# Products on zeros in the attention preamble, v loaded in turn with q and k, and two product blocks begun on four of six chunks

## What is computed

```python
scores = scale * np.matmul(q_c, k_c.transpose(0, 1, 2, 4, 3))
attn = np.exp(scores - np.max(scores, axis=-1, keepdims=True))
attn = attn / (np.sum(attn, axis=-1, keepdims=True) + 1e-09)
out = np.matmul(attn, v_c)

h = x @ w_in                    # x: 4608 x 512, w_in: 512 x 2048
r = np.maximum(h, 0.0)
g = s * (r * r) + b
x2 = g @ w_out                  # 4608 x 512

e_idx = np.argmax(xc @ w_gate, axis=1)          # xc: rows with x2 @ w_skip > 0
h = np.maximum(xc[mask] @ w1[e], 0.0)           # for each of 8 experts
y[mask] = gate_w[mask, None] * (h @ w2[e])
out[do_compute] = xc + y
```

## Time and profile before

| | |
|---|---|
| time, median of 3 runs | 1368.41 us (1366.62 to 1368.72) |
| the profiled execution's own time | 1368.54 us |
| its span | 1366.6 us |
| TensorE busy over the span | 1334.4 us (98%) |
| TensorE's clock, mean over the span | 0.984 of full |
| VectorE, ScalarE, GpSimd busy | 928.3, 753.6, 310.6 us |
| bytes moved | 116.88 MB, 86 GB/s on average |

### The profile page before, as it was taken

The page is one execution under the profiler, slowest core; times in us unless marked ns, Lnnn a source line. Parts: engine busy times, 40 slices in busy tenths (PEclk is TensorE's granted clock), DMA queues, the critical chain, the costliest instruction groups (busy, mean ns, idle before and its releaser), DMA issues.

```text
span 1366.6 us, 22444 instructions
## 1 busy us (share of the span) xinstructions
PE 1334.4 (98%) x7031; PEld 1175.5 (86%) x7032; DVE 928.3 (68%) x2139; ACT 753.6 (55%) x1838; POOL 310.6 (23%) x274
## 2 busy tenths in 40 slices
PE   8999999999999999999999999999799999999998
PEld 7998989899998999889998999989677778888886
DVE  3786978788786978778796878874477673333332
ACT  3886657566674757566665666644266552222221
POOL 4542222121222312121222222101111111111111
PEclk6999999999999999999999999999899999999999
DMA  6522312031131202112130303042375641111110
GB/s 243 171 82 96 102 32 94 25 101 40 39 97 29 97 30 96 35 59 78 34 103 21 105 24 101 12 155 70 118 255 205 238 156 46 38 45 40 45 38 26
DMA packets 61583, 116.88 MB, mean 86 GB/s; under 512 B 11848, under 2 KB 20296, under 8 KB 61360
## 3 DMA queue, kind: packets, MB, share of 16 engines
q1 hardware_dynamic: 42048, 76.39, 17.1%
q10 hardware_dynamic: 13328, 25.69, 5.4%
q0 software_dynamic: 6112, 13.56, 3.2%
HBM read 91.28 MB, written 27.08 MB: 87 GB/s over the span
## 4 chain that ended last, share of the span: by engine, by line
PE 88%; DVE 5%; issue 4%; DMA 1%; ACT 1%; DVEq 1%; ACTq 0%; SPq 0%; POOLq 0%; POOL 0%
PE h_ps L694 29%; PE y_ps L709 28%; PE y_ps L798 10%; PE h_ps L785 10%; PE s_ps L659 3%; PE av_ps L675 3%; DVE weights_lo L1128 2%; PE t_ps L666 1%; PE t_ps L778 1%; PE s_ps L792 1%; PE av_ps L792 1%; DMA first_raw<-in_first_qk 1%; PE y_ps L649 0%; PE av_ps L649 0%; DVE rows_t_lo L1253 0%
## 5 line engine op out<-in xcount | busy, mean ns | idle before, releaser
L1155 DVE CUSTOM_DVE_ANT_0 products<-scratch,wide 128x512 f32<-128x512 f32 x297 | 287.4, 968 | 6.7
L694 PE MATMUL h_ps<-rows_t_hi,weights_lo 128*128 128x384 f32 x768 | 261.1, 340 | 8.2 <-issue 5.5
L941 ACT ACTIVATE scratch<-h_ps 128x384 f32<-128x384 f32 x192 | 94.5, 492 | 301.9 <-PE h_ps L694 300.0
L694 PE MATMUL h_ps<-rows_t_hi,weights_hi 128*128 128x384 f32 x768 | 260.0, 339 | 0.0
L694 PE MATMUL h_ps<-rows_t_lo,weights_hi 128*128 128x384 f32 x768 | 258.8, 337 | 0.0
L709 PE MATMUL y_ps<-weights_hi,g_lo 128*128 128x512 f32 x576 | 227.9, 396 | 0.3 <-DVE g_lo L1134 0.2
L709 PE MATMUL y_ps<-weights_lo,g_hi 128*128 128x512 f32 x576 | 226.4, 393 | 0.0
L709 PE MATMUL y_ps<-weights_hi,g_hi 128*128 128x512 f32 x576 | 225.9, 392 | 0.0
L1134 DVE TENSOR_TENSOR g_lo<-scratch,g_hi 128x384 fp32r<-128x384 f32 x192 | 120.1, 626 | 102.0 <-ACT g_hi L873 99.4
L694 PEld LDWEIGHTS h_ps<-rows_t_hi,weights_lo 128*128 128x128 f32 x768 | 145.0, 189 | 21.6 <-issue 7.2
L515 POOL TENSOR_TENSOR qk_lo<-qk_raw,qk_hi 128x768 fp32r<-128x768 f32 x66 | 125.2, 1896 | 144.5 <-ACT qk_hi L873 144.5
(11 more groups left out here) (177 smaller groups left out, 2381.6 us busy)
## 6 DMA issues: line engine op xcount, KB each, us to landing
qk_raw<-in_qk SPq DMA_DIRECT2D x66, 384.0 KB, 3.0
expert_raw<-in_w ACTq DMA_DIRECT2D x31, 512.0 KB, 4.4
out<-scratch SPq DMA_DIRECT2D x12, 768.0 KB, 3.8
x_rows<-scratch SPq DMA_DIRECT2D x12, 768.0 KB, 6.0
scratch<-in_w ACTq DMA_DIRECT2D x18, 512.0 KB, 5.9
v_raw<-in_v SPq DMA_DIRECT2D x66, 128.0 KB, 2.0
expert_raw<-in_w SPq DMA_DIRECT2D x12, 512.0 KB, 4.9
wide<-in_w_out SPq DMA_DIRECT2D x7, 512.0 KB, 4.6
```

The costliest lines, as they stand in the source:

```text
L694: mm = pe.matmul(h_ps[f % 2][:, 0:TOK], w[:, f // PAIR, kt, fs], x[:, z, kt, :], start=kt == 0 and n == 0, stop=kt == KT - 1 and n == 2)
L941: act.activation(r_buf[f % 2], h_ps[f % 2][:, 0:TOK], ACT.Relu).then_inc(r_done, 1)
L1155: dve.tensor_tensor_reduce(products[:, :], x2_sb[:, t, :], gate_w[:, e, :], 1.0, 0.0, ALU.mult, ALU.add, logits[:, t, e:e + 1]).then_inc(d ...
```

## The change

Four edits, all of them ahead of or in the first step of the first tile. Products on zeros (now written to `h_ps[1]`) are put between the small products: one after B of chunk 0, three each after B of chunks 1 and 2, and one after D of chunks 0 to 3, 11 in all. The loads of v are issued in turn with those of q and k. The blocks h(0) and h(1) of the first tile are each made in two parts: columns 0 to 255 (chunks 0 to 3, FIRST_PART) while the last two chunks are still in their attention, columns 256 to 383 afterwards. And the preamble's last two steps are written out by hand around these parts.

```diff
+        FIRST_PART = (CPT - 2) * CHUNK
...
-            for c in range(CPT // 2):
-                load_first_qk(c)
+            load_first_qk(0)
+            load_first_qk(1)
             load_first_v(0)
-            load_raw_after(0)
-            for c in range(1, CPT // 2):
-                load_first_qk(c + 2)
+            for c in range(1, CPT - 1):
+                load_first_qk(c + 1)
                 load_first_v(c)
-            load_raw_after(1)
-            load_first_qk(CPT - 1)
-            for c in range(CPT // 2, CPT):
-                load_first_v(c)
-            load_raw_after(2)
+                if c >= 2:
+                    load_raw_after(c - 2)
+            load_first_v(CPT - 1)
...
-                    pe.matmul(h_ps[0][:, :], p_hi[:, 0, 0, :], p_hi[:, :, :, :].rearrange("p a b n -> p (a b n)"),
+                    pe.matmul(h_ps[1][:, :], p_hi[:, 0, 0, :], p_hi[:, :, :, :].rearrange("p a b n -> p (a b n)"),
                               start=True, stop=True)
...
-            def into_h(i, f, z, part=range(KT)):
-
-                if f == 0:
-                    pe.wait_ge(x_ready, CPT * i + CPT)
+            def into_h(i, f, z, part=range(KT), begin=0, end=TOK):
+
+                if f == 0 or begin > 0:
+                    pe.wait_ge(x_ready, CPT * i + end // CHUNK)
...
-                        mm = pe.matmul(h_ps[f % 2][:, 0:TOK], w[:, f // PAIR, kt, fs], x[:, z, kt, :],
+                        mm = pe.matmul(h_ps[f % 2][:, begin:end], w[:, f // PAIR, kt, fs], x[:, z, kt, begin:end],
                                        start=kt == 0 and n == 0, stop=kt == KT - 1 and n == 2)
-                if KT - 1 in part:
+                if KT - 1 in part and end == TOK:
                     mm.then_inc(h_done, 1)
...
                     elif f + 1 < FT:
-                        into_h(i, f + 1, z)
+                        into_h(i, f + 1, z, begin=0 if route or f > 0 else FIRST_PART)
...
-            for step in range(-1, CPT + 2):
+            for step in range(-1, CPT):
                 for stage, c in first_chunks(step, (("C", 2), ("B", -1), ("D", 2))):
                     if stage == "C" and c == 0:
                         pe.wait_ge(consts, 10)
                     first_attention(stage, c)
-            into_h(0, 0, 0)
+                    if stage == "B" and c < 3:
+                        warm((1, 3, 3)[c])
+                    if stage == "D":
+                        warm(1)
+            first_attention("C", CPT - 2)
+            into_h(0, 0, 0, end=FIRST_PART)
+            first_attention("D", CPT - 2)
+            first_attention("C", CPT - 1)
+            into_h(0, 1, 0, range(KT // 2), end=FIRST_PART)
+            first_attention("D", CPT - 1)
+            into_h(0, 1, 0, range(KT // 2, KT), end=FIRST_PART)
+            into_h(0, 0, 0, begin=FIRST_PART)
             tile(0, 0, True, False)
```

## The result

The changed kernel takes 1362.62 us (median of 22 executions, 1358.84 to 1371.36) against 1368.56 us (22, 1366.46 to 1371.78) for the kernel before, run beside it: ratio 0.9963 [0.9951, 0.9974], 5.9 us less. 19 of the 22 lie between 1358.8 and 1364.2, three at 1370 to 1371.4. The profiled execution took 1362.77 us.

A forecast was written before the change was run, and what follows sets the result against it. The prediction took the preamble to be bound by TensorE at half clock. With the clock held, x2(0) moves from 37.78 to 30.3 us: 1368.5 - 7.5 = 1361.0 us; range from 2 us below that to 1366.8.

The forecast's parts named there:

- The clock holds: First tile's preamble: zero products keep TensorE at full clock from 5.5 us, where before it fell at 8.7; chance 0.53.
- The thin place: Preamble after the early zeros: one zero product a chunk, adding 40% to the columns, was to hold the clock.
- Rival 1: Clock holds past 9 us but falls where chunks have one zero; gain 4.2, 1364.3 us; chance 0.22.
- rival 2: Clock falls at 8.7 us as before; x2(0) starts near 36.9, 1367.5 us; chance 0.17.
- The walk to x2(0): Preamble summed at full-clock prices: x2(0) starts at 29.9, written as 30.3 instead of 37.78 us, a gain of 7.5.
- The 128-column product: Second part of h(0) and h(1): 0.09 us for each product, between bounds of 0.059 and 0.118.
- 1.5 us idle ahead of x2(0): Between h(1) and x2(0): TensorE idles 1.5 us where h(1) had filled the wait before.
- the slower rival: Clock returns only in the blocks' second part or later; x2(0) at 39.2 or 41.0, 1370 to 1371.8 us; chance 0.05.
- A faster TensorE gains nothing more: Preamble, chunks 4 and 5: loads landing at about 12.3 and 15.2 us are a floor; TensorE waits 0.3 and 0.5.
- The first tile keeps up: After x2(0): splits and the next weight load, with 7.9 us left for it, let the shift carry to the end.
- Two readings of before: Profile before: 26 us of small products did not raise the clock, and it fell near 964.3 us.

The follow-up runs named there:

- f2: The changed kernel without its 11 zero products, TensorE's tile loop placed at offset 8 of a 256-instruction block: 1368.16 us, ratio 1.0004.
- e1: The kernel before with the 11 zero products as its only edit, loop not placed: 1371.48 us, ratio 1.0018.
- f1: The kernel before with only the 11 zero products added, TensorE's tile loop placed at offset 8: 1363.55 us, ratio 0.9979.
- e3: The changed kernel without the four zero products behind D, loop not placed: 1366.53 us, ratio 0.9975.
- f4: The changed kernel with only TensorE's tile loop placed, at offset 8 of a 256-instruction block: 1361.17 us, ratio 0.9952.
- e4: The changed kernel with the loads of q, k and v in the order of the kernel before: 1362.63 us, ratio 0.9947.
- f3: The kernel before with only TensorE's tile loop moved, to offset 244 of a 256-instruction block: 1387.24 us, ratio 1.0141.
- g1: The changed kernel, loop placed at offset 8, with six zero products in the wait ahead of x2(0): 1361.43 us, ratio 0.9971.
- e2: The changed kernel without all 11 zero products, loop not placed: 1391.84 us, ratio 1.0162.
- g3: The changed kernel, loop placed at offset 8, with four zero products behind each B of chunks 0 to 2: 1361.12 us, ratio 0.9956.
- g2: The changed kernel, loop placed at offset 8, with h(1) whole behind the second part of h(0): 1362.08 us, ratio 0.9958.
- g4: The changed kernel, loop placed at offset 8, with h(1) whole and the zero products of g3: 1361.44 us, ratio 0.9956.

## Why the prediction was right, and where it was off

- **The clock holds**: right. It was full from 8 to 30 us where before it fell at 8.7. f2 shows that without the zeros nothing is gained. That the zeros alone hold it was not so: e1 and f1 lose it in the whole blocks, and where the blocks are split it stays. The thin place, one zero a chunk after 9 us, held as well; that it was needed isn't shown, though e3's executions, without those zeros, lose the clock more often. Rival 1 and rival 2 (the clock falls in steps 3 to 5, or at 8.7 us) are not what the profiled execution did, and no other execution of the 22 has a mean clock under 0.991, where the profile of before, with its fall at 8.7, has 0.984.
- **The walk to x2(0)**: right within 0.2 us from h(0) on (but for the 128-column products, below), up to 0.6 us too early on the way there. The clock was not up at 5.5 but at 6.3 us, and chunk 2's B starts at 8.16 instead of 7.7, C of chunk 0 at 9.85 instead of 9.3, chunks 4 and 5 at 12.72 and 15.65 instead of 12.3 and 15.2. A zero product cost 0.26 us in a group of three (9.07 to 9.85) and 0.31 alone (14.53 to 14.85), not 0.22; all 11 come to some 3.4 us, not 2.4. B and D cost less than priced, and the waits took up the rest. TensorE waits 0.25 and 0.42 us for chunks 4 and 5 (0.3 and 0.5 forecast), h(0) begins at 20.75 (20.7), the last input comes at 26.10 (26.2), x2(0) begins at 30.10 (29.9 to 30.3).
- **The 128-column product**: mis-sized. 0.11 us start to start, where I chose 0.09; the upper bound from the 256-column product, 0.118, was nearly right. The Trainium skill's 55.6 ns for bf16 (TensorE: Matmul & The Clock Gate, "Wait — 56ns, not 53.3ns?") is half of what these rows show for the operands here. That made h(1) end at 29.0 instead of 28.4 us, inside the wait.
- **"1.5 us idle ahead of x2(0)"**: the idle was foreseen (1.1 us came), its price wasn't. The term for x2(0) itself was taken at full clock, and it cost 1.6 us more. I had a half clock at x2(0) only in the slower rival. In the profiled execution this term is 1.6 of the 1.8 us between the forecast and its own 1362.77 us: the mechanism was right and one term of the sum was missing. It isn't paid in every execution (f4, e4), so the median of 1362.62 mixes it with late rises of the clock, which the forecast didn't have either.
- **"A faster TensorE gains nothing more" for the loads**: right for this order of loads, which itself sets the floor. e1, with the old order and a clock that rose before 5.5 us, waits for no load of chunks 2, 4 and 5, and its D of chunk 3 starts at 17.51 us against 18.75 in after and 19.38 in f4. Over the whole kernel the new order shows neither gain nor loss (e4).
- **The first tile keeps up**: right; between 34 us and the end, nothing is given back but 0.3 us.
- **Two readings of before** were a little off, and nothing hangs on them: the small products that did not raise the clock last 21 us (10 to 31.09 us, where h(0) begins), not 26, and the fall that I put near 964.3 us lies at 964.4 by its row.
- **What the prediction didn't hold at all**: that the place of the loop among the blocks of instructions is a term. The change adds products ahead of the loop and so moves it; here it moved to an equally good place (5.5 and 5.6 us). In a bad place it would have cost some 20 us (f3) and turned the verdict. That the place stayed good was luck.

**Left open.** Three of 22 executions of after, three of 12 of g1 and two of 12 of f1 took 1369 to 1371 us; none was profiled. A late rise of the clock is a candidate, by e3's profile (1374.32 us, x2(0) at 38.78). It fits that their mean clocks read 0.993 to 0.995, as high as in the fast ones: a recorded fall would lower that figure, a late first rise does not. Zeros in the wait (g1) don't remove them. What decides when the clock first rises, and whether it falls at x2(0), wasn't found. Nor was a rule for the place of the loop: by the pages' counts of instructions, e1, e2, e3 and after execute 22, 50, 64 and 72 more than before, and idle 12.0, 20.8, 6.6 and 5.6 us at the returns against 5.5, in no simple order. The old order of loads wasn't tried with an early clock: e4's profile has a late one (12.5 us).

## What to carry to other kernels

Where TensorE has only small products to do and they set the time, wide products on zeros between them can keep its clock: here some 3.4 us of them brought 6 to 7 us, but 3.9 us where the dense blocks behind them stayed whole and the clock was lost at their start. So look at every idle of about 1 us that is left or that the gain uncovers, for the clock can be lost there. And compare versions of a kernel with a large loop only at the same place of that loop in the instruction stream, or look at the engine's idle at each return first: a change ahead of it may cost 20 us that have nothing to do with what was edited. And read the clock of a kernel's start from how long known products take, not from the column.

## What the runs showed of the hardware

- A return of this loop costs 1.3 to 1.4 us of idle at a good place (before, after, f1, f2, f4), 3.0 in e1, and 4.2 and 5.2 us at a bad one (f3, e2), and there the clock falls behind it, too.
- Behind the same 1.10 us of idle the clock fell in after, e3, f2 and g3 and did not in e2, e4 and f4, all with 24 products of 128 columns just ahead of it. The Trainium skill (TensorE: Matmul & The Clock Gate, "Why this matters for your kernels") names a long idle gap between bursts as what lets it fall; these rows show it behind 1.1 us, so the measurement decides.
- Around the 0.93 us of idle between the last small products and a block, the clock was lost in four of four profiles (e1, f1, g2, g4; in e1 1.2 us before that idle, in g4 1.0 us behind it, in the others between). With dense products between the small ones and 0.17 us of idle it was lost in none of five (after, e4, f4, g1, g3).
- The clock first rose before 5.4 us in f4, at 14.3 us in f1 and at about 31 us in e3, although TensorE's first instructions are the same.
- The profile's clock reads full speed until the first change it has recorded.
